# The first slot's sources worked out from one expert's ranks, gathered ahead of the other slots, in a fused attention and mixture-of-experts kernel

## The chip, the cores and the metric

One core of one Trainium2 chip. The metric is the device time of one execution in microseconds; lower is better. All times inside the kernel are microseconds from the first instruction of the profiled execution.

## The reference

Three stages, each feeding the next.

```python
# 1: attention, 2 batches x 8 heads, 768 rows, 64 columns; a row sees the columns of its own hash bucket
mask = q_bucket[:, :, :, None] == k_bucket[:, :, None, :]
scores = np.where(mask, scale * q @ k.T, -1e9);  attn = softmax(scores) @ v
x = attn.transpose(0, 2, 1, 3).reshape(1536, 512)
# 2: top-1 mixture of 8 experts, 512 -> 1024 -> 512
e_idx = np.argmax(x @ w_gate, axis=1)
gate_w = probs[np.arange(N), e_idx];  eom = sigmoid(x @ w_output_gate)
for e in range(8):
    ye = relu(x[e_idx == e] @ w1[e]) @ w2[e]
    out[e_idx == e] = gate_w * eom[:, e] * ye
# 3: dense layer, 512 -> 2048 -> 512, with ELU between
h = x @ w_in;  g = where(h > 0, h, exp(min(h, 0)) - 1);  return g @ w_out
```

## The kernel before

Attention comes first; its rows x are stored to DRAM (`x_rows`). Then the 1536 tokens are sorted by expert into 19 **slots** of 128 rows; every expert's rows start at a slot boundary. For each slot GpSimd gathers 128 rows of x with one indirect DMA (`gather_x`, 256 KB), TensorE turns them (`turn_x`), and runs layer 1, a turn of the hidden rows (`turn_h`) and layer 2 with the expert's weights. Stage 3 follows.

Each engine has its own list of instructions, written out by hand; semaphores tie the lists together. On the vector engine `then(...)` makes the next instruction wait for the one in it. What matters here is the stretch from the end of attention (about 243 us) to layer 1 of slot 1 (263 us):

- **Ranks.** TensorE sums the one-hot matrix of the experts into `ring[0]` (`s_rank`). The ranks are each token's place within its expert, and the counts of all experts.
- **Places.** The vector engine turns ranks into a row number for each token (`c_up`, `c_full`, `s_cum`, `r_b`, `r_at`, `r_tile`, `r_low`), then into two one-hot tensors: `place` (which slot) and `at_row` (which of the 128 rows; three instructions of 4 tiles each, L1048).
- **Sources.** Twelve matmuls of `at_row` and `place` (L1426) give the token number of every row of every slot (`s_token`). The vector engine copies them to `src` (L1054, `s_src`), and GpSimd starts the gathers (L607).
- **Slot table and gates.** The vector engine then works out `slot_tab` (which expert and which of two weight buffers a slot uses: L1055 to L1062, `s_tab`) and the gates' values (L1065 to L1073, `s_parts`). GpSimd multiplies these into `place_g` (L618), for 12 matmuls that TensorE runs behind layer 1 of slot 0 (`gates()`, L1500).
- **Slot 0.** TensorE reads `slot_tab` twice (`expert(0)`), turns the rows of slot 0 (L1441), the scalar and the vector engine copy them (`copy_xt(0)`), and layer 1 runs (L1475).
- **Row numbers.** Behind `copy_xt(0)` the vector engine works out `row_at` and `out_row` (L1144 to L1160). Only then does its loop over the slots begin: `relu(0)` (L1100), `copy_xt(1)` (L1091), and so on.
- **TensorE behind layer 1 of slot 0:** `gates()`, `expert(1)`, `turn_x(1)`, `turn_h(0)` (L1450, waits for `relu(0)`), layer 1 of slot 1.
- **Filling.** `warm(i)` runs WARM[i] matmuls of 512 columns without a use (L1401), so that TensorE is not idle while it waits.
- **Weights.** Expert 1's weights (8 transfers of 512 KB, SyncE, L500) are issued when the rows of slot 0 have landed (`s_xld[0]`). The scalar engine rounds them (L756) and GpSimd works out the low parts (`w_lo`, L518). GpSimd's list is: gathers 0 to 3, the two `place_g`, gathers 4 and 5, then in turn one `w_lo(1, c)` and one gather, eight times.

## Time and profile before

| what | value |
|---|---|
| median of 3 runs (lowest, highest) | 769.1 us (768.97, 769.7) |
| the profiled execution's own time | 769.18 us |
| its span, first to last instruction | 767.4 us |
| TensorE busy | 755.5 us, 98% of the span |
| VectorE, ScalarE, GpSimd busy | 423.9, 345.1, 368.6 us |
| mean granted TensorE clock | 0.997 of full speed |

The span is 1.78 us shorter than the execution's own time. TensorE is busy for nearly all of it, but busy also covers the filling matmuls, so what counts is when real work starts.

### The profile page before, as it was taken

The page shows a single profiled execution, that of the slowest core. Times are in us where ns is not written, and L with a number is a line of the kernel's source. Part 1 is how long each engine was busy: PE and PEld are TensorE (multiplying, and loading weights), DVE is VectorE, ACT ScalarE, POOL GpSimd, SP SyncE. Part 2 cuts the span into 40 slices and gives each one's busy share as a digit, 9 for nine tenths or more (in the row PEclk, how much of TensorE's full clock was granted, in tenths as well). Part 3 has the DMA queues.
Part 4 walks back from the last instruction along what each step waited for, and adds up shares of the span by engine and source line. Part 5 has one row for each costly group of instructions (what it writes and reads, how often), then busy time and mean ns, then how long its engine had stood idle before and what let it go on. Part 6 is the DMA issues. An engine that isn't in the chain of part 4 may idle for free.

```text
span 767.4 us, 12551 instructions
## 1 busy us (share of the span) xinstructions
PE 755.5 (98%) x4247; PEld 631.2 (82%) x4247; DVE 423.9 (55%) x844; ACT 345.1 (45%) x656; POOL 368.6 (48%) x253
## 2 busy tenths in 40 slices
PE   8899999999999999999999999999999999999996
PEld 7677777777776788888888888998899889989985
DVE  8777777777765645454444445588147126414710
ACT  7766677777764214432244210185047117404610
POOL 4776567878720799777987870244200120010001
PEclk9999999999999999999999999999999999999998
DMA  4534323212111867655675610520100010000000
GB/s 100 123 111 107 105 76 94 68 49 67 27 46 26 295 227 261 208 190 166 224 237 164 239 55 28 185 105 1 57 26 1 28 56 1 0 28 15 1 14 28
DMA packets 42781, 73.70 MB, mean 96 GB/s; under 512 B 20352, under 2 KB 24096, under 8 KB 42720
## 3 DMA queue, kind: packets, MB, share of 16 engines
q1 hardware_dynamic: 29632, 30.05, 13.4%
q10 hardware_dynamic: 9584, 31.53, 12.4%
q0 software_dynamic: 3504, 11.30, 4.5%
q8 instruction: 38, 0.62, 0.3%
q14 instruction: 23, 0.19, 0.1%
HBM read 60.48 MB, written 11.28 MB: 94 GB/s over the span
## 4 chain that ended last, share of the span: by engine, by line
PE 62%; issue 29%; POOL 4%; DVE 2%; ACT 1%; DMA 1%; SPq 0%; POOLq 0%; DVEq 0%
PE pair_s L1475 14%; PE pair_t L1490 14%; PE pair_u L1282 8%; PE bank_b L1297 8%; PE pair_s L1269 5%; PE pair_t L1269 4%; PE pair_u L1450 2%; PE bank_b L1321 1%; POOL out L646 1%; PE pair_s L1528 1%; DVE g_lo L1211 1%; PE pair_s L1401 1%; PE bank_a L1238 1%; POOL y_raw L640 1%; POOL w_part L518 1%
## 5 line engine op out<-in xcount | busy, mean ns | idle before, releaser
L518 POOL TENSOR_TENSOR w_part<-w_raw,w_part 128x1024 fp32r<-128x1024 f32 x80 | 190.3, 2405 | 57.5 <-ACT w_part L756 57.3
L756 ACT ACTIVATE w_part<-w_raw 128x1024 fp32r<-128x1024 f32 x72 | 73.7, 1054 | 125.4 <-PE pair_t L1490 99.8
L1577 PE MATMUL pair_t<-w_part,g_hi 128*128 128x512 f32 x384 | 119.0, 391 | 0.3 <-POOL w_part L518 0.3
L646 POOL DMA_INDIRECT out<-o_sb,token x12 | 11.8, 986 | 208.5 <-DVE o_sb L1181 208.5
L1475 PE MATMUL pair_s<-w_part,xs_t 128*128 x456 | 108.8, 394 | 0.2 <-issue 0.2
L1490 PE MATMUL pair_t<-w_part,hid_t 128*128 x456 | 109.0, 394 | 0.0
L1475 PEld LDWEIGHTS pair_s<-w_part,xs_t 128*128 128x128 f32 x456 | 84.3, 188 | 17.7 <-issue 0.9
L1490 PEld LDWEIGHTS pair_t<-w_part,hid_t 128*128 128x128 f32 x456 | 84.4, 188 | 16.8
L855 ACT ACTIVATE elu<-elu 128x384 f32<-128x384 f32 x64 | 33.6, 525 | 124.3 <-DVE elu L1201 124.1
L698 ACT ACTIVATE exps<-exps,nmax 128x768 f32<-128x768 f32 x96 | 88.5, 926 | 1.1 <-DVE exps L912 1.0
L1282 PEld LDWEIGHTS pair_u<-first,exps 128*128 128x128 f32 x564 | 64.3, 140 | 24.2 <-issue 19.0
L1577 PEld LDWEIGHTS pair_t<-w_part,g_hi 128*128 128x128 f32 x384 | 71.6, 188 | 15.1 <-issue 0.7
L1282 PE MATMUL pair_u<-first,exps 128*128 128x128 f32 x564 | 80.7, 277 | 1.8 <-ACT exps_t L706 0.9
L941 DVE COPY exps_t<-pair_u 128x384 f32<-128x384 f32 x94 | 52.1, 554 | 42.6 <-PE pair_u L1282 42.3
L1577 PE MATMUL pair_t<-w_part,g_lo 128*128 128x512 f32 x192 | 74.9, 390 | 0.0
L706 ACT ACTIVATE exps_t<-pair_u 128x384 f32<-128x384 f32 x94 | 45.9, 488 | 59.9 <-PE pair_u L1282 59.3
L1528 PE MATMUL pair_u<-y_t,w_part 128*128 128x384 f32 x384 | 69.3, 334 | 0.3 <-DVE elu L1206 0.3
L1528 PE MATMUL pair_s<-y_t,w_part 128*128 128x384 f32 x384 | 69.3, 335 | 0.0
L1528 PEld LDWEIGHTS pair_u<-y_t,w_part 128*128 128x128 f32 x384 | 66.8, 188 | 0.7 <-DVE elu L1206 0.6
L1528 PEld LDWEIGHTS pair_s<-y_t,w_part 128*128 128x128 f32 x384 | 66.9, 188 | 0.2
L1109 DVE CAST hid_t<-pair_u 128x512 fp32r<-128x512 f32 x38 | 26.0, 685 | 67.2 <-PE pair_u L1450 67.2
L1297 PE MATMUL bank_b<-exps_t,v_nat 128*64 128x384 f32 x336 | 60.4, 495 | 0.0
(219 smaller groups left out, 1091.8 us busy)
## 6 DMA issues: line engine op xcount, KB each, us to landing
w_raw<-in_moe_w ACTq DMA_DIRECT2D x48, 512.0 KB, 6.3
w_raw<-in_moe_w SPq DMA_DIRECT2D x16, 512.0 KB, 5.8
ys_sorted<-ys SPq DMA_DIRECT2D x19, 256.5 KB, 3.7
w_raw<-in_moe_w_in ACTq DMA_DIRECT2D x8, 512.0 KB, 5.2
raw<-in_q SPq DMA_DIRECT2D x16, 192.0 KB, 3.2
raw<-in_k SPq DMA_DIRECT2D x16, 192.0 KB, 3.4
v_nat<-in_v SPq DMA_DIRECT2D x16, 192.0 KB, 2.6
x_rows<-rows_sb SPq DMA_DIRECT2D x32, 96.0 KB, 2.4
```

What stands on the lines that cost most here:

```text
L518: pool.tensor_tensor(chunk_of(w_part, n, 1, c), w_raw[n % 2][c][:, :], chunk_of(w_part, n, 0, c).bitcast(F32), ALU.subtract).then_inc(s_wl ...
L698: act.activation(exps[:, m % 4, :], exps[:, m % 4, :], ACT.Exp, scale=-1.0, bias=nmax[:, g % 2, qt:qt + 1], accum_out=den[:, u % 4, qt:qt ...
L706: act.activation(turned_tile(m, slice(0, JH)), exps_pair(m)[:, 0, 0:HALF].rearrange("p (j n) -> p j n", j=JH), ACT.Copy).then_inc(s_t0, 1)
L756: act.activation(chunk_of(w_part, n, 0, c), w_raw[n % 2][c][:, :], ACT.Copy).then_inc(s_whi, 1)
L941: dve.tensor_copy(turned_tile(m, slice(JH, J)), exps_pair(m)[:, 1, 0:HALF].rearrange("p (j n) -> p j n", j=JH)).then_inc(s_t1, 1)
L1269: mm = pe.matmul(score_pair[m % 2][:, h, 0:HALF], a[rows, g % 3, t], b[rows, g % 3, h * HALF:(h + 1) * HALF], start=first, stop=not first)
L1282: mm = pe.transpose(exps_pair(m)[:, part, n * P:(n + 1) * P], exps[:, m % 4, kt * P:(kt + 1) * P], ident)
L1297: mm = pe.matmul(u_bank(u)[o * D:(o + 1) * D, 0:HALF], v_nat[:, (u - 1 + o) % 4, j, :], turned_half(2 * u - 1 + o)[:, j], start=j == 0, st ...
L1475: mm = pe.matmul(pair_s[:, h, :], xs_t[:, xp, c * P:(c + 1) * P], w_part[:, bass.ds(par, 1), wp, a:a + 512], start=c == 0 and xp == 0 and ...
L1490: mm = pe.matmul(pair_t[:, s % 2, :], hid_t[:, hp, c * P:(c + 1) * P], w_part[:, bass.ds(par, 1), wp, a:a + DM], start=c == 0 and n == 0, ...
L1528: mm = pe.matmul(hidden_bank[n % 4][:, 0:NB], w_in_p[:, wp, c, f * P:(f + 1) * P], y_t[:, yp, c, :], start=c == 0 and m == 0, stop=c == CD ...
L1577: mm = pe.matmul(pair_t[:, t % 2, :], gp[:, f, j * P:(j + 1) * P], w_out_p[:, wp, f, :], start=f == 0 and m == 0, stop=f == FT - 1 and m == 2)
```

## The change

A second way to the sources is added for slot 0, which belongs to expert 0 whatever the data are. `r_first` is the rank within expert 0, less 1024 for tokens of that expert. Compared with a constant row `lowered` (0 to 127, less 1024), it gives `at_row` for slot 0 alone. Twelve matmuls with the token numbers (`row_two`, made on the scalar engine) give the first column of `src`, and gather 0 waits for that (`s_srcf`) and not for `s_src`. The way of before follows, for all slots; the block between `e_cmp` and the second `gate_part` (L1055 to L1073) is moved word for word. The slot table and the gates' arithmetic stand behind `copy_xt(0)`. TensorE no longer reads the slot table for slot 0: its expert and its buffer are constants. The filling matmuls are 10, 4, 12, 3 in place of 10, 14, 16, 3.

```diff
-WARM = (10, 14, 16, 3)
+WARM = (10, 4, 12, 3)
+APART = 1024.0
+    put("lowered", np.arange(P) - APART)
@@ gpsimd
-            pool.wait_ge(s_src, 1)
+            pool.wait_ge(s_srcf, 1)
             for i in range(2):
                 pool.wait_ge(s_xst[i], 16 * HEADS)
-            for s in range(FIRST_SLOTS):
+            gather_x(0)
+            pool.wait_ge(s_src, 1)
+            for s in range(1, FIRST_SLOTS):
                 gather_x(s)
@@ scalar
             act.activation(r_z[:, :], r_z[:, :], ACT.Exp, scale=-1.0).then_inc(s_rb, 1)
+            act.activation(row_two[:, :, :], cc("row").unsqueeze(2).broadcast_to([P, TILES, 2]), ACT.Copy).then_inc(s_two, 1)
@@ vector
+            then(dve.scalar_tensor_tensor(r_first[:, :], oh[:, :, 0], -APART, rank[:, 0:TILES, 0], ALU.mult, ALU.add))
+            for t in range(0, TILES, AT):
+                dve.tensor_tensor(at_row[:, t:t + AT, :], cc("lowered").unsqueeze(1).broadcast_to([P, AT, P]),
+                                  r_first[:, t:t + AT].unsqueeze(2).broadcast_to([P, AT, P]),
+                                  ALU.is_equal).then_inc(s_atf, 1)
             then(dve.tensor_scalar(c_up[:, :], rank[:, TILES, :], 1.0, float(P - 1), ALU.max, ALU.add))
...
+            dve.wait_ge(s_first, 1)
+            dve.tensor_copy(src[:, 0:1], ring[2][:, 0:1]).then_inc(s_srcf, 1)
...
             dve.wait_ge(s_token, 1)
-            dve.tensor_copy(src[:, :], ring[1][:, 0:SLOTS]).then_inc(s_src, 1)
+            dve.tensor_copy(src[:, 1:SLOTS], ring[1][:, 1:SLOTS]).then_inc(s_src, 1)
-            then(dve.tensor_tensor(e_cmp[:, :, :], s_cum[:, 1:E].unsqueeze(1).broadcast_to([P, SLOTS, E - 1]),
...
-            dve.tensor_tensor(gate_part[:, 1, :], gate[:, :], gate_part[:, 0, :].bitcast(F32),
-                              ALU.subtract).then_inc(s_parts, 1)
...
             copy_xt(0)
+
+            then(dve.tensor_tensor(e_cmp[:, :, :], s_cum[:, 1:E].unsqueeze(1).broadcast_to([P, SLOTS, E - 1]),
...
+            dve.tensor_tensor(gate_part[:, 1, :], gate[:, :], gate_part[:, 0, :].bitcast(F32),
+                              ALU.subtract).then_inc(s_parts, 1)
@@ tensor
             warm(1)
+            pe.wait_ge(s_two, 1)
+            for t in range(TILES):
+                if t % AT == 0:
+                    pe.wait_ge(s_atf, t // AT + 1)
+                mm = pe.matmul(ring[2][:, 0:2], at_row[:, t, :], row_two[:, t, :], start=t == 0, stop=t == TILES - 1)
+                if t % AT == AT - 1 and t < TILES - 1:
+                    pe.matmul(pair_s[:, 0, 0:P], w_part[:, 0, 1, 0:P], w_part[:, 0, 0, 0:P], start=True, stop=True)
+            mm.then_inc(s_first, 1)
+            warm(2)
...
-            warm(2)
-            pe.wait_ge(s_tab, 1)
             pe.wait_ge(s_cnt, 1)
             pe.wait_ge(s_src, 1)
-            of = {0: expert(0)}
+            of = {0: (0, NC1, NCH)}
             turn_x(0)
             warm(3)
...
                 if s == 0:
                     gates()
+                    pe.wait_ge(s_tab, 1)
```

On the vector engine, right behind the wait for the ranks, this stood before (the first rows of the chain that ends in `r_low`):

```order
L1030 TENSOR_SCALAR c_up<-bank_a 128x8 [waits s_rank]
L1031 TENSOR_SCALAR c_full<-c_up 128x8 [waits s_dd]
L1032 SCALAR_TENSOR_TENSOR s_cum<-cst,c_full 128x8 [waits s_dd]
L1033 TENSOR_TENSOR r_b<-s_cum,bank_a 128x96 [waits s_dd]
L1035 TENSOR_TENSOR r_b<-r_b,onehot 128x96 [waits s_dd]
```

And this stands there now:

```order
L1038 SCALAR_TENSOR_TENSOR r_first<-onehot,bank_a 128x12 [waits s_rank]
L1040 TENSOR_TENSOR at_row<-cst,r_first 128x512 [waits s_dd]
L1040 TENSOR_TENSOR at_row<-cst,r_first 128x512 x2
L1043 TENSOR_SCALAR c_up<-bank_a 128x8
L1044 TENSOR_SCALAR c_full<-c_up 128x8 [waits s_dd]
L1045 SCALAR_TENSOR_TENSOR s_cum<-cst,c_full 128x8 [waits s_dd]
L1047 CAST src<-pair_u 128x1 [waits s_first,s_dd]
L1048 TENSOR_TENSOR r_b<-s_cum,bank_a 128x96
```

So the old chain from `r_b` on stands behind five added instructions and a wait for TensorE. On the same engine, behind the wait for the sources of all slots, this stood before:

```order
L1054 CAST src<-bank_b 128x19 [waits s_token]
L1055 TENSOR_TENSOR e_cmp<-s_cum,cst 128x133
L1057 TENSOR_TENSOR e_alt<-e_cmp,cst 128x133 [waits s_dd]
L1059 TENSOR_REDUCE tab_f<-e_alt 128x19 [waits s_dd]
L1060 TENSOR_REDUCE tab_f<-e_cmp 128x19
L1061 TENSOR_SCALAR tab_f<-s_cum 128x8
L1062 CAST slot_tab<-tab_f 128x46 [waits s_dd]
L1065 TENSOR_REDUCE r_p<-r_a 128x12 [waits s_rb]
```

And this stands there now:

```order
L1069 CAST src<-bank_b 128x18 [waits s_token]
L1076 CAST xs_t<-bank_b 128x256 [waits s_xt]
L1078 TENSOR_TENSOR xs_t<-bank_a,xs_t 128x256 [waits s_xta]
L1081 TENSOR_TENSOR xs_t<-bank_b,xs_t 128x256 [waits s_xte]
L1136 TENSOR_TENSOR e_cmp<-s_cum,cst 128x133
L1138 TENSOR_TENSOR e_alt<-e_cmp,cst 128x133 [waits s_dd]
L1140 TENSOR_REDUCE tab_f<-e_alt 128x19 [waits s_dd]
```

The 14 instructions from `e_cmp` to the second `gate_part` now stand between `copy_xt(0)` and `c_end`, the first of the 13 that work out the row numbers; `relu(0)` still stands behind those. On TensorE, from the last group of matmuls that give the sources, this stood before:

```order
L1426 MATMUL bank_b<-place,at_row 128x20 [waits s_at,s_place]
L1426 MATMUL bank_b<-place,at_row 128x20 x3
L1401 MATMUL pair_s<-w_part 128x512 x16
L1455 TENSOR_LOAD slot_tab [waits s_src,s_cnt,s_tab]
L1455 ISA x2
L1456 TENSOR_LOAD slot_tab
L1456 ISA x2
L1441 MATMUL bank_a<-first,xs_raw 128x128 [waits s_xld0]
```

And this stands there now:

```order
L1449 MATMUL bank_b<-place,at_row 128x20 [waits s_at,s_place]
L1449 MATMUL bank_b<-place,at_row 128x20 x3
L1464 MATMUL bank_a<-first,xs_raw 128x128 [waits s_xld0,s_src,s_cnt]
L1464 MATMUL bank_a<-first,xs_raw 128x128
L1464 MATMUL bank_b<-first,xs_raw 128x128 x2
L1415 MATMUL pair_s<-w_part 128x512 x3
```

The turn of slot 0's rows now stands right behind those matmuls, and still waits for the sources of all slots, since it writes over the bank that they are read from.

## Rows read from the trace of the kernel before

**Rows 1.** Busy time by stretch (from:to, length, busy of each engine, granted clock, DMA)
```profile
252.00:253.00 1.00, 0.82 (x4) 0.36 (x2) 0.73 (x4) 0.00 (x0) 0.78 (x1) 1.00 0.67 176
...
270.00:480.00 210.00, 210.00 (x1025) 177.18 (x1024) 100.76 (x155) 59.03 (x59) 157.47 (x75) 1.00 0.54 180
```
**Rows 2.** The chain that ended last, slot 0 (start, length, what)
```profile
249.55 3.47 DMA xs_raw<-x_rows,src
...
253.06 0.51 PE bank_a L1441 x2
...
254.59 5.75 PE pair_s L1475 x24
```
**Rows 3.** Timeline of DVE, ranks to sources (start, length, [idle before])
```profile
243.93 0.17 DVE L1030 TENSOR_SCALAR c_up<-bank_a 128x8 uint32<-128x8 f32 x1 [0.15 <-PE bank_a L1410]
...
244.55 0.26 DVE L1033 TENSOR_TENSOR r_b<-s_cum,bank_a 128x96 f32<-128x96 f32 x1
...
246.43 1.89 DVE L1048 TENSOR_TENSOR at_row<-cst,r_low 128x512 fp32r<-128x512 f32 x3
...
249.09 0.18 DVE L1054 CAST src<-bank_b 128x19 uint32<-128x19 f32 x1 [0.69 <-PE bank_b L1426]
```
**Rows 4.** Timeline of PE, the last group of source matmuls
```profile
248.46 0.58 PE L1426 MATMUL bank_b<-place,at_row 128*128 128x20 f32 x4
```
**Rows 5.** Timeline of DVE, from the sources to the copies of slot 1
```profile
249.18 0.29 DVE L1055 TENSOR_TENSOR e_cmp<-s_cum,cst 128x133 f32<-128x133 f32 x1
...
252.66 0.17 DVE L1073 TENSOR_TENSOR gate_part<-gate,gate_part 128x12 fp32r<-128x12 f32 x1
...
254.61 0.41 DVE L1088 TENSOR_TENSOR xs_t<-bank_b,xs_t 128x256 fp32r<-128x256 f32 x1
...
255.13 0.48 DVE L1145 TENSOR_TENSOR pad<-c_full,counts 128x8 f32<-128x8 uint32 x1
...
258.05 0.18 DVE L1160 TENSOR_TENSOR out_row<-part_f,tile_f 128x19 uint32<-128x19 f32 x1
...
260.45 1.22 DVE L1100 TENSOR_SCALAR hid<-pair_s 128x1024 f32<-128x1024 f32 x1 [2.22 <-PE pair_s L1475]
...
262.29 0.69 DVE L1091 CAST xs_t<-bank_b 128x512 fp32r<-128x512 f32 x1 [0.61 <-PE bank_b L1441]
```
**Rows 6.** Timeline of PE, behind layer 1 of slot 0
```profile
260.18 1.41 PE L1500 MATMUL pair_t<-place_g,at_row 128*128 128x40 f32 x12
261.43 0.75 PE L1441 MATMUL bank_b<-first,xs_raw 128*128 128x128 f32 x4
262.02 1.05 PE L1450 MATMUL pair_u<-first,hid 128*128 128x128 f32 x8
263.23 5.75 PE L1475 MATMUL pair_s<-w_part,xs_t 128*128 x24 [0.17 <-issue]
```
**Rows 7.** Timeline of PE, the same place one slot later
```profile
274.78 1.05 PE L1450 MATMUL pair_u<-first,hid 128*128 128x128 f32 x8
275.59 5.72 PE L1475 MATMUL pair_s<-w_part,xs_t 128*128 x24
```
**Rows 8.** Timeline of POOL: gather 0, place_g, first and fourth low part
```profile
249.55 1.09 POOL L607 DMA_INDIRECT xs_raw<-x_rows,src  x1 [14.60 <-DVE src L1054]
...
254.44 1.15 POOL L618 TENSOR_TENSOR place_g<-in_slot,gate_part 128x240 fp32r<-128x240 f32 x2
...
260.01 2.38 POOL L518 TENSOR_TENSOR w_part<-w_raw,w_part 128x1024 fp32r<-128x1024 f32 x1 [1.99 <-ACT w_part L756]
...
270.62 2.41 POOL L518 TENSOR_TENSOR w_part<-w_raw,w_part 128x1024 fp32r<-128x1024 f32 x1
```
**Rows 9.** DMA issues, us to landing: of 252 to 253, then 253.6 to 254.5
```profile
xs_raw<-x_rows,src POOLq DMA_INDIRECT x1, 5.6
...
xs_raw<-x_rows,src POOLq DMA_INDIRECT x1, 8.7
```
**Rows 10.** Timeline of SyncE's queue: expert 1's weights
```profile
253.09 4.78 SPq L500 DMA_DIRECT2D w_raw<-in_moe_w  x8
```

More of the change, by code:

```diff
@@ L92 @@
            ("twice", D), ("rev", TILES * E), ("slot", SLOTS * (E - 1)), ("starts", TILES * COLS),
-           ("alt", SLOTS * (E - 1)), ("iota", P), ("row", TILES)]
+           ("alt", SLOTS * (E - 1)), ("iota", P), ("lowered", P), ("row", TILES)]
 COL = {}
@@ L204, in program @@
             r_low = sb("r_low", [P, TILES])
+            r_first = sb("r_first", [P, TILES])
+            row_two = sb("row_two", [P, TILES, 2], F32R)
             lg_part = sb("lg_part", [P, J, 2 * E])
@@ L339, in program @@
         s_src = sem("s_src")
+        s_atf, s_first, s_srcf, s_two = sem("s_atf"), sem("s_first"), sem("s_srcf"), sem("s_two")
         s_wld = [sem(f"s_wld{c}") for c in range(NCH)]
@@ L1053, in _ @@
             dve.wait_ge(s_token, 1)
-            dve.tensor_copy(src[:, :], ring[1][:, 0:SLOTS]).then_inc(s_src, 1)
-            then(dve.tensor_tensor(e_cmp[:, :, :], s_cum[:, 1:E].unsqueeze(1).broadcast_to([P, SLOTS, E - 1]),
-                                   cc("slot").rearrange("p (s e) -> p s e", e=E - 1), ALU.is_le))
-            then(dve.tensor_tensor(e_alt[:, :, :], e_cmp[:, :, :],
-                                   cc("alt").rearrange("p (s e) -> p s e", e=E - 1), ALU.mult))
-            dve.tensor_reduce(tab_f[:, 0:SLOTS], e_alt[:, :, :], AX.X, ALU.add)
-            dve.tensor_reduce(tab_f[:, SLOTS:2 * SLOTS], e_cmp[:, :, :], AX.X, ALU.add)
-            then(dve.tensor_scalar(tab_f[:, 2 * SLOTS:], s_cum[:, 1:E + 1], 1.0 / P, 1.0, ALU.mult, ALU.add))
-            dve.tensor_copy(slot_tab[:, :], tab_f[:, :]).then_inc(s_tab, 1)
-            dve.wait_ge(s_rb, 1)
-            then(dve.tensor_reduce(r_p[:, :], r_a[:, :, :], AX.X, ALU.add))
-            then(dve.tensor_scalar(r_p[:, :], r_p[:, :], EPS, None, ALU.add))
-            then(dve.reciprocal(r_p[:, :], r_p[:, :]))
-            dve.wait_ge(s_rb, 2)
-            then(dve.tensor_scalar(r_z[:, :], r_z[:, :], 1.0, None, ALU.add))
-            then(dve.reciprocal(r_z[:, :], r_z[:, :]))
-            then(dve.tensor_tensor(gate[:, :], r_p[:, :], r_z[:, :], ALU.mult))
-            then(dve.tensor_copy(gate_part[:, 0, :], gate[:, :]))
-            dve.tensor_tensor(gate_part[:, 1, :], gate[:, :], gate_part[:, 0, :].bitcast(F32),
-                              ALU.subtract).then_inc(s_parts, 1)
+            dve.tensor_copy(src[:, 1:SLOTS], ring[1][:, 1:SLOTS]).then_inc(s_src, 1)
             def copy_xt(s):
@@ L1141, in _ @@
             copy_xt(0)
+            then(dve.tensor_tensor(e_cmp[:, :, :], s_cum[:, 1:E].unsqueeze(1).broadcast_to([P, SLOTS, E - 1]),
+                                   cc("slot").rearrange("p (s e) -> p s e", e=E - 1), ALU.is_le))
+            then(dve.tensor_tensor(e_alt[:, :, :], e_cmp[:, :, :],
+                                   cc("alt").rearrange("p (s e) -> p s e", e=E - 1), ALU.mult))
+            dve.tensor_reduce(tab_f[:, 0:SLOTS], e_alt[:, :, :], AX.X, ALU.add)
+            dve.tensor_reduce(tab_f[:, SLOTS:2 * SLOTS], e_cmp[:, :, :], AX.X, ALU.add)
+            then(dve.tensor_scalar(tab_f[:, 2 * SLOTS:], s_cum[:, 1:E + 1], 1.0 / P, 1.0, ALU.mult, ALU.add))
+            dve.tensor_copy(slot_tab[:, :], tab_f[:, :]).then_inc(s_tab, 1)
+            dve.wait_ge(s_rb, 1)
+            then(dve.tensor_reduce(r_p[:, :], r_a[:, :, :], AX.X, ALU.add))
+            then(dve.tensor_scalar(r_p[:, :], r_p[:, :], EPS, None, ALU.add))
+            then(dve.reciprocal(r_p[:, :], r_p[:, :]))
+            dve.wait_ge(s_rb, 2)
+            then(dve.tensor_scalar(r_z[:, :], r_z[:, :], 1.0, None, ALU.add))
+            then(dve.reciprocal(r_z[:, :], r_z[:, :]))
+            then(dve.tensor_tensor(gate[:, :], r_p[:, :], r_z[:, :], ALU.mult))
+            then(dve.tensor_copy(gate_part[:, 0, :], gate[:, :]))
+            dve.tensor_tensor(gate_part[:, 1, :], gate[:, :], gate_part[:, 0, :].bitcast(F32),
+                              ALU.subtract).then_inc(s_parts, 1)
             dve.wait_ge(s_cnt, 1)
```

## The prediction

> **What bounds the kernel now.** I read the busy time by stretch first. From 270 to 480 us TensorE is busy for the whole 210.00 us at full clock [rows 1]: from slot 1 on nothing makes it wait, so whatever moves the start of that stretch moves the end by as much. The question is only when TensorE begins layer 1 of slot 1, at 263.23 us [rows 6].
>
> The chain that ended last names what holds the stretch ahead of it. Gather 0 leaves at 249.55 us and takes 3.47 us to land; TensorE turns the rows at 253.06 us, 0.04 us after they are there, and layer 1 of slot 0 starts at 254.59 us [rows 2]. TensorE looks busy then, but with filling matmuls. Gather 0 waits for the sources, copied at 249.09 us, and those for a chain on the vector engine that starts with the ranks at 243.93 us [rows 3].
>
> The timelines of the vector engine and TensorE show the stretch up to slot 1. The vector engine has the slot table and the gates at 249.18 to 252.83 us (3.65 us, inside the gather's flight), and from its last copy of slot 0, L1088 at 254.61 us, to the end of L1160 at 258.23 us another 3.62 us. Then it stands idle 2.22 us until layer 1 ends, and starts `relu(0)` at 260.45 us [rows 5]. TensorE has the gates' matmuls, turns slot 1's rows at 261.43 us, the hidden rows at 262.02 us, and starts layer 1 at 263.23 us [rows 6]. From the turn of the hidden rows to the next layer 1 is 1.21 us here and 0.81 us one slot later [rows 7]: 0.40 us are a wait for L1091, which ends at 262.98 us [rows 5].
>
> **The change, step by step.**
>
> *The way for slot 0.* `r_first` is one more chained instruction of 12 elements; its like, three from 243.93 to 244.55 us, take 0.21 us each [rows 3]. The three new `at_row` have the shape of L1048: 1.89 us [rows 3]. They end at 243.93 + 0.21 + 1.89 = 246.03 us. In the way of before the last four matmuls ended 0.72 us after `at_row` (249.04 against 248.32 us) [rows 3, 4]; two columns in place of twenty cost between nothing and as much, and I take as much: 246.75 us. `c_up` to `s_cum` fill 0.62 us of that, so the vector engine waits 0.1 us. It copies column 0 at 246.80 us, against 249.09 us. The stores of x are not in the way: the gather waited for `src` alone [rows 8]. Gather 0 leaves 2.29 us earlier and lands at about 250.73 us. Making `row_two` on the scalar engine is priced by no row here; it lies beside the 2 us of `at_row`.
>
> *The way for all slots.* It is pushed back by what was put ahead of it: `r_b` stood at 244.55 us and comes at 246.89 us (0.09 us behind the copy, as L1055 behind L1054 [rows 3, 5]), 2.34 us later. The sources of all slots are copied at 251.43 to 251.61 us. The turn of slot 0's rows still waits for them. **So the gather is no longer what comes last; the pushed-back chain is.** With 0.14 us from the vector engine to TensorE (248.32 to 248.46 us [rows 3, 4]) the turn starts at 251.75 us: 1.31 us earlier than 253.06 us. Layer 1 of slot 0 moves from 254.59 to 253.28 us and ends at 259.03 us. The two reads of the slot table that are gone lay behind the wait for the gather; I count nothing for them. Queued behind the new waits are, on TensorE, 12 filling matmuls, which end before the sources come, and on GpSimd gathers 1 to 3, 0.9 us later than before.
>
> *The moved block.* It leaves a place where the gather's flight hid it and comes to one where layer 1 of slot 0 hides it, if it fits. L1088 starts at 254.61 - 1.31 = 253.30 us. Behind it stand 3.62 us as before and the block's 3.65 us: `relu(0)` can start at 260.57 us. Layer 1 ends at 259.03 us. The old slack of 2.22 us is 1.43 us too short for a block of 3.65 us, and this eats the 1.31 us: `relu(0)` starts about when it did (260.45 us). It ends at 261.79 us, and the turn of the hidden rows starts at about 261.95 us against 262.02 us. TensorE now stands still before it for about a microsecond, since its turn of slot 1's rows is over at 260.9 us.
>
> *What is left.* With slot 1's rows turned that early, their copy L1091 follows `relu(0)` at once and ends near 262.5 us. The wait of 0.40 us before layer 1 of slot 1 goes: it starts 0.81 us behind the turn of the hidden rows, at 262.76 us. That is 0.47 us earlier.
>
> *Two instructions at a time on VectorE and GpSimd.* L1145 works on 8 elements and takes 0.48 us, where L1160 with 19 takes 0.18 us; it ended at 255.61 us, as `place_g` did on GpSimd at 255.59 us [rows 5, 8]. So 0.30 us of the 3.62 us are a wait for GpSimd. In the new order `place_g` waits for the moved block and runs exactly beside the row numbers' arithmetic, which has several instructions with two inputs from SBUF. The cost is between nothing (0.30 us less than before) and the whole 1.15 us of the two `place_g` (0.85 us more) [rows 8]. I take 0.15 us more, nearer to the row. The Trainium skill (SBUF — State Buffer, "Who interferes with whom") says that a VectorE instruction with two SBUF inputs contends with a GpSimd instruction that reads SBUF, and that the one that started first holds the ports for its whole length. The trace agrees in L1145; by the rule taken strictly, the sum would be near the upper end just given.
>
> *Sum.* -0.07 us (turn of the hidden rows) - 0.40 us (wait that goes) + 0.15 us = -0.3 us. The profiled execution took 769.18 us, 0.08 us over the median of the runs; 769.1 - 0.3 = 768.8 us.
>
> **What is hidden.** GpSimd starts `place_g` at about 257.4 us and not 254.44 us, is through at 258.6 us, and TensorE wants it at 259.0 us or somewhat earlier; were it late by 1 us, TensorE's wait for `relu(0)` would still cover it. Behind come two gathers, of 1.09 us and some 0.2 us between, and then `w_lo(1, 0)` at 261.2 us in place of 260.01 us: 1.2 us later. Layer 1 of slot 2, the first of expert 1, needs four of them; the fourth ended at 270.62 + 2.41 = 273.03 us [rows 8] and would end at 274.2 us, against a start of that layer at 275.59 us [rows 7], or 275.1 us with the gain. This cover of 0.9 us is gone if the vector engine's block runs a microsecond longer, and then it costs what it exceeds it by.
>
> **The rivals.**
>
> *The gain passes whole.* If `relu(0)` were ready by 259.1 us, layer 1 of slot 1 would start 1.31 us earlier: 767.8 us. It needs the vector engine's 7.27 us between L1088 and `relu(0)` to shrink by 1.4 us. Against it: these are the block's own measured lengths, and no more than 0.3 us of waiting in the 3.62 us is seen in the rows. Partial shrinking is likelier.
>
> *Contention at its upper end.* `place_g` holds up the row numbers for 0.85 us more: +0.4 us, 769.5 us.
>
> *Gather 1 comes late; the slower side.* It leaves at 251.61 + 0.28 = 251.9 us. Expert 1's weights, 4 MB, used to be issued at 253.09 us [rows 10], behind gather 1; now they are issued when gather 0 lands, at 250.8 us, ahead of it. The gather issued at 252.22 us took 5.6 us, one among the weights 8.7 us [rows 9]. By these gather 1 lands between 257.5 and 260.6 us, and TensorE wants it at 260.1 us. It decides only beyond 261.2 us, since the turn of the hidden rows waits until 261.95 us. With a landing after 10.7 us the turn of slot 1's rows would start at 262.7 us and layer 1 of slot 1 at 264.2 us: +1.0 us, 770.1 us.
>
> *Slot 0 does not start earlier.* The added way costs more than the 2.34 us, as by 1.3 us, and the turn of slot 0's rows stands where it did. Then `relu(0)` comes 1.3 us later than forecast: 770.1 us. Against it: every added step has its like in rows 3.
>
> **How the numbers follow.** Forecast (between 0.8 us less and 0.1 us more): 0.66. Gain whole: 0.12. Contention: 0.10. Gather 1 late: 0.07. No earlier start: 0.05. The likeliest is 768.8 us. The range goes from the whole gain to most of the way to the two slow cases: 767.7 to 769.9 us. A measurement of this kernel can tell about 0.2%, 1.54 us. Faster than 767.56 us needs more than the whole gain: 0.05. Slower than 770.64 us needs a slow case beyond its price: 0.04. Within: 0.91.
>
> **What would show it.** Gather 0 issued near 247.3 us, the turn of slot 0's rows near 251.8 us right behind the copy of the sources and not the landing, and the granted clock 1.00 there, as it is where TensorE was busy 0.82 of a microsecond [rows 1]. `relu(0)` near 260.6 us with the vector engine never idle before it, TensorE idle about 1 us before the turn of the hidden rows, no wait before layer 1 of slot 1, which starts at 262.8 to 263.1 us. A vector engine that is idle before `relu(0)` would prove me wrong on the main step; TensorE waiting for the DMA of slot 1's rows, on the gather.

## The result, and the profile after

The changed kernel takes 773.08 us in the median of 5 runs (772.4 to 773.61), the kernel before 769.1 us (768.97 to 769.7, 5 runs): ratio 1.005, 95% interval 1.004 to 1.0061. It is slower by about 4 us. The profiled execution took 772.98 us, with a span of 771.2 us against 767.4 us.

The vector engine from the ranks to `relu(0)`, as a timeline (start, length, line, operation, [idle before]); it answers to [rows 3] and [rows 5]:

```profile
243.77 0.17 DVE L1038 SCALAR_TENSOR_TENSOR r_first<-onehot,bank_a 128x12 f32<-128x12 bf16 x1 [0.15 <-PE bank_a L1424]
...
246.64 0.16 DVE L1047 CAST src<-pair_u 128x1 uint32<-128x1 f32 x1 [0.27 <-PE pair_u L1436]
...
251.24 0.17 DVE L1069 CAST src<-bank_b 128x18 uint32<-128x18 f32 x1 [0.69 <-PE bank_b L1449]
...
253.50 0.29 DVE L1136 TENSOR_TENSOR e_cmp<-s_cum,cst 128x133 f32<-128x133 f32 x1
...
256.58 0.17 DVE L1154 TENSOR_TENSOR gate_part<-gate,gate_part 128x12 fp32r<-128x12 f32 x1
...
256.88 0.58 DVE L1159 TENSOR_TENSOR pad<-c_full,counts 128x8 f32<-128x8 uint32 x1
257.49 0.61 DVE L1160 TENSOR_TENSOR past<-cst,c_end 128x96 f32<-128x96 f32 x1
...
259.54 0.18 DVE L1171 CAST tile_f<-tile_no 128x19 f32<-128x19 uint32 x1
259.75 3.05 DVE L1172 SCALAR_TENSOR_TENSOR part_f<-part_f,tile_f 128x19 f32<-128x19 f32 x1
262.83 0.17 DVE L1173 TENSOR_SCALAR tile_f<-tile_f 128x19 f32<-128x19 f32 x1
263.04 0.18 DVE L1174 TENSOR_TENSOR out_row<-part_f,tile_f 128x19 uint32<-128x19 f32 x1
263.25 1.22 DVE L1093 TENSOR_SCALAR hid<-pair_s 128x1024 f32<-128x1024 f32 x1
```

Down to L1171 it runs as forecast or a little ahead; the ranks were there at 243.77 us and not at 243.93 us, so 0.16 us of that lead is not the change's. Then one instruction of 19 elements, L1172, takes 3.05 us where its neighbours take 0.18 us. `relu(0)` (L1093) stands behind it and starts at 263.25 us, not at 260.45 us as before [rows 5]. GpSimd at the same time, against [rows 8]:

```profile
247.08 1.14 POOL L612 DMA_INDIRECT xs_raw<-x_rows,src  x1 [12.29 <-DVE src L1047]
...
256.84 1.15 POOL L625 TENSOR_TENSOR place_g<-in_slot,gate_part 128x240 fp32r<-128x240 f32 x2 [1.68 <-DVE gate_part L1154]
...
259.42 0.95 POOL L612 DMA_INDIRECT xs_raw<-x_rows,src  x1 [0.30 <-issue]
260.39 2.37 POOL L523 TENSOR_TENSOR w_part<-w_raw,w_part 128x1024 fp32r<-128x1024 f32 x1
```

L1172 ends at 262.80 us, 0.04 us after the first low part, `w_lo(1, 0)` (L523), at 262.76 us. In the kernel before, that low part began at 260.01 us, when the row numbers had been over since 258.23 us [rows 5, 8]: the two never met. TensorE's timeline, against [rows 6] and [rows 2]:

```profile
251.52 0.48 PE L1464 MATMUL bank_a<-first,xs_raw 128*128 128x128 f32 x2 [0.32 <-issue]
...
253.46 6.52 PE L1498 MATMUL pair_s<-w_part,xs_t 128*128 128x512 f32 x24
259.81 1.41 PE L1523 MATMUL pair_t<-place_g,at_row 128*128 128x40 f32 x12
261.07 0.75 PE L1464 MATMUL bank_b<-first,xs_raw 128*128 128x128 f32 x4
264.53 1.16 PE L1473 MATMUL pair_u<-first,hid 128*128 128x128 f32 x8 [2.72 <-DVE hid L1093]
265.45 7.34 PE L1498 MATMUL pair_s<-w_part,xs_t 128*128 x24
```

The turn of slot 0's rows is 1.54 us earlier than before, and the turn of the hidden rows 2.51 us later, after a wait of 2.72 us for `relu(0)`. Layer 1 of slot 1 then takes 7.34 us in place of 5.75 us. The reason stands in the busy times by stretch (from:to, length, busy of each engine, granted clock, DMA share, GB/s), against [rows 1]:

```profile
252.00:253.00 1.00, 1.00 (x4) 0.84 (x4) 0.58 (x2) 0.38 (x1) 0.69 (x2) 0.50 0.70 217
...
260.00:264.00 4.00, 1.81 (x15) 1.62 (x15) 3.90 (x4) 2.12 (x2) 3.80 (x4) 1.00 1.03 407
...
265.00:266.00 1.00, 1.00 (x9) 0.91 (x8) 0.93 (x4) 0.86 (x1) 1.00 (x1) 0.80 1.01 414
266.00:269.00 3.00, 3.00 (x9) 2.32 (x8) 2.61 (x4) 2.12 (x2) 2.82 (x3) 0.50 0.65 242
...
270.00:480.00 210.00, 210.00 (x1024) 177.12 (x1023) 100.38 (x153) 56.91 (x56) 157.78 (x75) 1.00 0.54 178
```

TensorE was busy 1.81 of 4 us from 260 to 264 us, and from 266 to 269 us its granted clock is 0.50: 1.2 GHz in place of 2.4 GHz. A first fall stands at 252 us, where TensorE is recorded as busy all the time. From 270 us on there is no wait, as before. So the loss is whole by then: layer 1 of slot 1 starts 2.2 us late and takes 1.6 us longer, which is the 3.8 us of the spans.

### The profile page after: what moved, and what is told of

It reads as the page before. It is cut to its first block, busy times and chain, and to the rows that moved or that the text cites. A ratio compares the mean times of both kernels' runs of the same rounds, so it can differ in the third digit from the quotient of the medians.

```text
span 771.2 us, 12520 instructions
## 1 busy us (share of the span) xinstructions
PE 757.0 (98%) x4247; PEld 632.8 (82%) x4247; DVE 428.6 (56%) x849; ACT 345.2 (45%) x657; POOL 368.5 (48%) x253
## 4 chain that ended last, share of the span: by engine, by line
PE 61%; issue 29%; DVE 4%; POOL 4%; ACT 1%; DMA 1%; SPq 0%; POOLq 0%; DVEq 0%
PE pair_t L1513 14%; PE pair_s L1498 13%; PE pair_u L1296 8%; PE bank_b L1311 8%; PE pair_s L1283 4%; PE pair_t L1283 4%; PE pair_u L1473 2%; PE bank_b L1335 1%; POOL out L653 1%; PE pair_s L1549 1%; DVE g_lo L1225 1%; PE pair_s L1415 1%; PE bank_a L1252 1%; POOL y_raw L647 1%; POOL w_part L523 1%
## 5 line engine op out<-in xcount | busy, mean ns | idle before, releaser
L523 POOL TENSOR_TENSOR w_part<-w_raw,w_part 128x1024 fp32r<-128x1024 f32 x80 | 190.1, 2401 | 59.1 <-ACT w_part L763 58.9
L1498 PE MATMUL pair_s<-w_part,xs_t 128*128 (+1 forms) x456 | 111.2, 401 | 0.0
L1513 PE MATMUL pair_t<-w_part,hid_t 128*128 (+1 forms) x456 | 109.0, 395 | 0.0
L1498 PEld LDWEIGHTS pair_s<-w_part,xs_t 128*128 128x128 f32 x456 | 86.3, 192 | 17.7
```

What stands on the lines that cost most here:

```text
L523: pool.tensor_tensor(chunk_of(w_part, n, 1, c), w_raw[n % 2][c][:, :], chunk_of(w_part, n, 0, c).bitcast(F32), ALU.subtract).then_inc(s_wl ...
L1498: mm = pe.matmul(pair_s[:, h, :], xs_t[:, xp, c * P:(c + 1) * P], w_part[:, bass.ds(par, 1), wp, a:a + 512], start=c == 0 and xp == 0 and ...
L1513: mm = pe.matmul(pair_t[:, s % 2, :], hid_t[:, hp, c * P:(c + 1) * P], w_part[:, bass.ds(par, 1), wp, a:a + DM], start=c == 0 and n == 0, ...
```

## The experiments

All kernels here compute the whole reference. The theory was the **hold** (theory L): L1172 is kept from ending by the first low part, and the wait that follows lets the clock fall. The rivals were the clock alone (theory C), a slow L1172 for a reason of its own (theory O), the length of the moved block itself, and the added way for slot 0. Each diff is against the changed kernel where the text names no other, and shows the lines that matter; a line of dots stands for what is left out. e1 to e12 are the names of the experiments.

**The low part behind the row numbers** (e1). `w_lo(1, 0)` waits for `out_row`; a copy of one element signals it.

```diff
+            pool.wait_ge(s_outrow, 1)
             for c in range(NCH):
                 w_lo(1, c)
```

> The changed kernel, with one wait more: GpSimd begins the first low part of expert 1's weights only when the vector engine has written out_row. In the changed kernel L1172, a scalar_tensor_tensor of 19 elements with two inputs from SBUF, took 3.05 us and ended at 262.80 us, 0.04 us after that low part (260.39 to 262.76 us) ended on GpSimd. Theory L (VectorE was held up by GpSimd's low part, 2.7 us of the 3.8 us lost): L1172 takes about 0.2 us, relu(0) starts at 260.4 to 260.7 us in place of 263.25 us, TensorE waits under 1 us before the turn of the hidden rows, and the time is 769 to 770.5 us. Theory C (TensorE's clock is what costs: it fell to half in 252 to 255 us and in 265 to 269 us): the two falls stay, at least the first, and the time stays above 771 us even if relu(0) is early. Theory O (L1172 is slow for a reason of its own, its place in the program or its data): it takes 3 us again, and the time stays at 773 us.

Measured: 769.03 us, ratio to the kernel before 1.0003 (0.9994 to 1.0013). The vector engine's timeline of this kernel:

```profile
259.75 0.18 DVE L1174 SCALAR_TENSOR_TENSOR part_f<-part_f,tile_f 128x19 f32<-128x19 f32 x1
259.97 0.40 DVE L1175 TENSOR_SCALAR tile_f<-tile_f 128x19 f32<-128x19 f32 x1
260.40 0.18 DVE L1177 TENSOR_TENSOR out_row<-part_f,tile_f 128x19 uint32<-128x19 f32 x1
...
260.68 1.22 DVE L1095 TENSOR_SCALAR hid<-pair_s 128x1024 f32<-128x1024 f32 x1
```

The same instruction at the same 259.75 us takes 0.18 us, so it is not slow by itself. The low part begins at 260.85 us. Layer 1 of slot 1 starts at 263.09 us. The whole 4.05 us between the changed kernel and this one come from the low part's place. The first fall of the clock was there too (0.59 from 252 to 256 us), so it isn't part of the loss.

**The row numbers of the output later** (e2). `part_row` to `out_row` stand behind `copy_ht(0)`.

```diff
-            then(dve.tensor_scalar(part_row[:, :], src[:, :], P - 1, None, ALU.bitwise_and))
...
                 copy_ht(s)
+                if s == 0:
+                    out_rows()
```

> The changed kernel, with the seven instructions from part_row to out_row behind copy_ht(0), so that only c_end to row_at stand ahead of relu(0). Theory L: relu(0) is no longer behind the held instruction and starts when layer 1 of slot 0 ends, 259.1 to 260.0 us; layer 1 of slot 1 starts at 262.0 to 262.6 us, and the seven instructions may each be held by a low part further on, beside TensorE's work, without a cost. Time 768 to 769.5 us, 767.5 to 768 us if the clock does not fall. Theory C: relu(0) is early, but the clock still falls in 252 to 255 us, which costs about 1 us: 769 to 770 us. Theory O (the slow instruction is slow anywhere): a 3 us instruction stands behind copy_ht(0), where it costs nothing, so the same times as by L; only its length tells them apart, if it does not lie beside a low part.

Measured: 769.26 us, ratio 1.0003 (0.9993 to 1.0012). `relu(0)` starts at 258.67 us and layer 1 of slot 1 at 261.79 us, 1.44 us earlier than before [rows 6]. But the moved instructions now meet the second, third and fourth low part:

```profile
265.05 1.17 DVE L1169 TENSOR_SCALAR part_row<-src 128x19 uint32<-128x19 uint32 x1
...
266.67 3.09 DVE L1172 CAST tile_f<-tile_no 128x19 f32<-128x19 uint32 x1
...
270.22 3.09 DVE L1175 TENSOR_TENSOR out_row<-part_f,tile_f 128x19 uint32<-128x19 f32 x1
```

The low parts run from 263.76 to 266.17 us, 267.31 to 269.72 us and 270.85 to 273.27 us, and each held instruction ends within 0.05 us of one. `relu(1)` stands behind all three and starts at 273.35 us, and TensorE waits 1.2 us for it. So the hold goes with the pair of instructions that meet, not with the place in the program.

**The moved block alone** (e3; the diff is against the kernel before). The kernel before, with the block behind `copy_xt(0)` and slot 0's constants, without the way for slot 0.

```diff
             copy_xt(0)
+            then(dve.tensor_tensor(e_cmp[:, :, :], s_cum[:, 1:E].unsqueeze(1).broadcast_to([P, SLOTS, E - 1]),
...
-            of = {0: expert(0)}
+            of = {0: (0, NC1, NCH)}
```

> The kernel before, with one part of the change alone: the slot table and the gates' arithmetic behind copy_xt(0), and TensorE's constants for slot 0. No second way for slot 0, the fillings as before (10, 14, 16, 3). L1088 stays at 254.6 us, and behind it stand 3.62 + 3.65 us: relu(0) at 261.9 us if nothing holds the vector engine, 1.4 us later than before; with it layer 1 of slot 1 starts 1.0 to 1.3 us later: 770.1 to 770.5 us. Theory L: an instruction of the row numbers may be caught beside a low part or a gather of GpSimd again; each caught costs up to 2.4 us: 770.5 to 773 us. Theory C: with the old fillings the clock does not fall before slot 0 (PEclk 1.00 in 252 to 255 us); a second fall behind a long wait would show a granted clock of 0.5 in 264 to 270 us.

Measured: 774.52 us, ratio 1.0075 (1.0058 to 1.0091). The hold is there (3.03 us from 261.24 us, low part from 261.87 us), TensorE waits 4.0 us, and the clock falls to 0.70 from 264 to 268 us.

**The moved block alone, low part behind the row numbers** (e6). The diff is against e3; `out_row` signals `s_outrow`.

```diff
+            pool.wait_ge(s_outrow, 1)
             for c in range(NCH):
                 w_lo(1, c)
```

> The kernel before with the moved block alone, as in the run at 774.5 us, and GpSimd's first low part of expert 1 behind out_row. Theory L: the 3.03 us of L1158 become about 0.2 us, relu(0) starts at about 262.0 us in place of 264.7 us, TensorE waits about 1.2 us and not 4.0 us, the clock does not fall, and layer 1 of slot 1 starts at about 264.3 us, 1.1 us later than before: 770.2 us (770 to 771). The rest over the kernel before is the block itself. If the hold were not what cost in that run, the time stays over 773 us.

Measured: 770.08 us, ratio 1.0013 (1.0004 to 1.0022); TensorE waits 1.3 us and the clock stays at 1.00. So of the 5.4 us of e3 about 1 us is the block's own length in its new place, and 4.4 us are the hold and the clock.

**The way for slot 0 alone** (e4). The changed kernel, with the block in front of `copy_xt(0)`.

```diff
             dve.tensor_copy(src[:, 1:SLOTS], ring[1][:, 1:SLOTS]).then_inc(s_src, 1)
+            then(dve.tensor_tensor(e_cmp[:, :, :], s_cum[:, 1:E].unsqueeze(1).broadcast_to([P, SLOTS, E - 1]),
...
             copy_xt(0)
```

> The changed kernel, with the slot table and the gates' arithmetic back where they were, ahead of copy_xt(0); the second way for slot 0 and the fillings 10, 4, 12, 3 stay. The sources are copied at 251.4 us, the block ends at 255.1 us, so the copies of slot 0 come 2.6 us later than in the changed kernel, layer 1 of slot 0 starts at about 256.0 us (1.4 us later than before), and relu(0) is ready for it. Theory L: no instruction of the vector engine of over 1 us before relu(0); time 770 to 771 us with a full clock. Theory C: the clock falls near 252 us in this kernel too, since the sparse matmuls ahead are the same, and costs 0.8 to 1.5 us more: 771 to 772.5 us.

Measured: 774.52 us, ratio 1.0066 (1.004 to 1.0091). I had expected no hold, and this failed: two instructions are held, by two low parts. The vector engine, and then GpSimd:

```profile
258.52 2.97 DVE L1171 CAST tile_f<-tile_no 128x19 f32<-128x19 uint32 x1
...
261.95 3.06 DVE L1174 TENSOR_TENSOR out_row<-part_f,tile_f 128x19 uint32<-128x19 f32 x1
```

```profile
259.04 2.41 POOL L523 TENSOR_TENSOR w_part<-w_raw,w_part 128x1024 fp32r<-128x1024 f32 x1
...
262.59 2.38 POOL L523 TENSOR_TENSOR w_part<-w_raw,w_part 128x1024 fp32r<-128x1024 f32 x1
```

GpSimd, done with `place_g` sooner, begins its low parts sooner (259.04 us in place of 260.01 us), since expert 1's weights come sooner: they are issued at 250.93 us in place of 253.09 us, and the first low part no longer waits for the scalar engine's rounding [rows 8, 10]. Either half of the change brings the row numbers and the low parts together: the block by pushing the first back, the way for slot 0 by pulling the second forward, and here the row numbers are 1.25 us later as well (`part_row` at 257.86 us in place of 256.61 us). The holds aren't the whole of this kernel's loss: its layer 1 of slot 0 waits for the copies and starts at 255.52 us, 0.93 us later than before, and the clock is at 0.51 from 252 to 256 us and at 0.72 from 264 to 268 us.

**The wait filled** (e5). The changed kernel, with 10 filling matmuls of 512 columns in front of the turn of slot 0's hidden rows. It tells the clock from the wait.

```diff
+                if s == 0:
+                    for i in range(10):
+                        pe.matmul(pair_t[:, 0, :], w_part[:, 0, 1, 0:P], w_part[:, 0, 0, 0:512], start=True, stop=True)
                 if s < SLOTS:
                     turn_h(s)
```

> The changed kernel, with ten filling matmuls of 512 columns on TensorE between the turn of slot 1's rows and the turn of slot 0's hidden rows, where it waited 2.7 us for relu(0). The vector engine's held instruction stays. If the wait is what lets the clock fall behind it (granted clock 0.5 in 265 to 269 us of the changed kernel, where layer 1 of slot 1 took 7.3 us), the clock stays at 1.00 there, that layer takes 5.75 us, and the time is about 1.3 us less than the changed kernel's 773.1: 771.5 to 772 us. If the fall has another cause, layer 1 of slot 1 takes 7 us again and the time stays at 773 us.

Measured: 771.45 us, ratio 1.0034 (1.0022 to 1.0046). The hold is unchanged (3.06 us). Its stretches:

```profile
252.00:256.00 4.00, 4.00 (x14) 3.12 (x13) 3.34 (x14) 1.71 (x3) 2.70 (x3) 0.59 0.94 329
...
264.00:268.00 4.00, 3.81 (x22) 3.10 (x21) 3.86 (x8) 2.46 (x3) 3.83 (x3) 1.00 0.82 331
```

The first fall stays, the second is gone, and layer 1 of slot 1 takes 5.70 us. The second fall is worth 773.08 - 771.45 = 1.6 us, the hold the other 771.45 - 769.03 = 2.4 us.

**Wider fillings between the source matmuls** (e10). The changed kernel, with the four single fillings between the groups (two among the matmuls for slot 0, two among those for all slots) 512 columns wide and not 128. One of the two places:

```diff
-                    pe.matmul(pair_s[:, 0, 0:P], w_part[:, 0, 1, 0:P], w_part[:, 0, 0, 0:P], start=True, stop=True)
+                    pe.matmul(pair_s[:, 0, :], w_part[:, 0, 1, 0:P], w_part[:, 0, 0, 0:512], start=True, stop=True)
```

> The changed kernel, with 512 columns in place of 128 in the four single filling matmuls between the groups of source matmuls. The clock's first fall (granted clock 0.5 in 252 to 255 us) does not come: layer 1 of slot 0 takes 5.7 us and not 6.5 us. The held instruction and the second fall behind it stay. Since relu(0) waits for the vector engine and not for layer 1, the time moves little: 772.5 to 773.5 us by theory L. If the first fall is part of the 4 us lost, it is 771.5 to 772.3 us.

Measured: 772.92 us, ratio 1.0049 (1.0033 to 1.0064). The clock is 1.00 from 252 to 256 us and layer 1 of slot 0 takes 5.72 us, but TensorE only waits longer for `relu(0)`: 4.0 us. The second fall stays. The first fall costs nothing as long as the hold is there.

**The low part in four pieces** (e9). The changed kernel, `w_lo(1, 0)` as four instructions of 256 columns.

```diff
+                    for i in range(4):
+                        at = slice(i * CHUNK // 4, (i + 1) * CHUNK // 4)
+                        done = pool.tensor_tensor(chunk_of(w_part, 1, 1, 0)[:, at], w_raw[1][0][:, at],
+                                                  chunk_of(w_part, 1, 0, 0)[:, at].bitcast(F32), ALU.subtract)
```

> The changed kernel, with the first low part of expert 1's weights (one GpSimd instruction of 1024 columns, 2.38 us) as four instructions of 256 columns. In the changed kernel L1172 on the vector engine took 3.05 us, from 0.3 us into gather 5 to the end of that low part. Theory L, with the hold lasting as long as the GpSimd instruction that is running (and not as long as GpSimd is busy): the instruction is freed after the first piece, 0.6 to 0.7 us instead of 2.38 us, so it takes 1.2 to 1.5 us, and those behind it may each be held for one piece: relu(0) starts at 261.5 to 262.7 us in place of 263.25 us, and the time is 770.5 to 772.5 us. If the vector engine is held as long as GpSimd has work of any kind, L1172 takes 3 us again and the time stays at 773 us. Theory O: the same, 3 us and 773 us.

Measured: 770.39 us, ratio 1.003 (1.0016 to 1.0043). The vector engine, and GpSimd's four pieces:

```profile
259.75 0.79 DVE L1180 SCALAR_TENSOR_TENSOR part_f<-part_f,tile_f 128x19 f32<-128x19 f32 x1
260.58 0.64 DVE L1181 TENSOR_SCALAR tile_f<-tile_f 128x19 f32<-128x19 f32 x1
261.25 0.66 DVE L1182 TENSOR_TENSOR out_row<-part_f,tile_f 128x19 uint32<-128x19 f32 x1
```

```profile
260.37 2.81 POOL L635 TENSOR_TENSOR w_part<-w_raw,w_part 128x256 fp32r<-128x256 f32 x4
```

One hold of 3.05 us became three of 0.64 to 0.79 us, where one piece takes 0.72 us, and `relu(0)` starts at 261.95 us. A hold goes by the GpSimd instruction, not by how long GpSimd has work: that was without a pause from 260.37 to 263.18 us. I had expected the first hold to last until the first piece ends, 1.2 to 1.5 us; it was over at 260.54 us, 0.17 us after that piece's record begins. The Trainium skill (SBUF — State Buffer, "Who interferes with whom") says that the engine that comes second is blocked for the first one's whole instruction; the rows agree on the length. They don't agree on the order: by the records the vector instruction begins first (259.75 us against 260.39 us in the changed kernel), and still it is the one that waits.

**Better versions** (e7, e8, e11, e12). The diff of e7 is against the changed kernel, those of e11 and e12 are against e8. The question was whether the earlier start can reach the end at all. In e7 the first four instructions of the output rows stand right behind the copy of the sources, in idle time, and GpSimd's gathers 4 and 5 and the low parts wait for `out_row`:

```diff
             dve.tensor_copy(src[:, 1:SLOTS], ring[1][:, 1:SLOTS]).then_inc(s_src, 1)
+            dve.wait_ge(s_src, 1)
+            then(dve.tensor_scalar(part_row[:, :], src[:, :], P - 1, None, ALU.bitwise_and))
...
+            pool.wait_ge(s_outrow, 1)
             for s in range(FIRST_SLOTS, NEXT_SLOTS):
                 gather_x(s)
```

> The changed kernel with two edits: the first four of the seven instructions of out_row stand right behind the copy of src, in the 0.9 us in which the vector engine waits for the turn of slot 0's rows; and GpSimd begins gathers 4 and 5 and the first low part only when out_row is written. Theory L: nothing holds the vector engine for more than 0.6 us before relu(0), which starts at 259.0 to 259.6 us; layer 1 of slot 1 starts at 261.8 to 262.2 us, 1.0 to 1.4 us earlier than before, no instruction of the vector engine stands beside a low part afterwards that TensorE waits for, and the gain stays to the end: 767.7 to 768.1 us with a full clock, up to 769.2 us in executions in which the clock falls near 252 us. If the moved start is lost somewhere further on in any case, 769 us.

Measured: 768.75 us, ratio 0.9999 (0.999 to 1.0008), with the clock at 0.58 from 252 to 256 us, layer 1 of slot 0 at 6.91 us and layer 1 of slot 1 from 263.13 us. No instruction is held any more, but I had expected that layer from 261.8 to 262.2 us: `relu(0)` now waits 0.94 us for the slow layer 1 of slot 0. e8 adds the wide fillings of e10:

> The kernel with split rows, and the four single filling matmuls between the groups of source matmuls with 512 columns in place of 128. If the clock falls near 252 us because TensorE had little to stream in 244 to 251 us, it falls in fewer executions or not at all: the median is at or below that of the kernel with split rows, by up to 1 us, and the spread of its times is narrower. The wider fillings may push the sources back by 0.1 to 0.3 us. If the fall has nothing to do with it, the median is 0 to 0.3 us higher and the spread is the same.

Measured: 769.19 us, ratio 1.0005 (0.9996 to 1.0014). The clock stays at 1.00 and layer 1 of slot 1 starts at 262.17 us, 1.06 us earlier than before. The time isn't at or below e7's, as I had expected with the clock up. TensorE's waits show where it is lost:

```profile
PE pair_s L1502 <- POOL w_part L524: 0.9, 1, 0.9
```

Layer 1 of slot 2 waits for the fourth low part of expert 1, which is over at 275.43 us, not at 273.03 us. e11 puts the low parts in front of gathers 4 and 5 and leaves two gathers for the end of the list:

```diff
-            for s in range(FIRST_SLOTS, NEXT_SLOTS):
-                gather_x(s)
...
                 w_lo(1, c)
-                gather_x(NEXT_SLOTS + c)
+                gather_x(FIRST_SLOTS + c)
+            for s in range(FIRST_SLOTS + NCH, NEXT_SLOTS + NCH):
+                gather_x(s)
```

> The kernel with split rows and wide fillings, and with another order on GpSimd: the first low part stands right behind out_row and gathers 4 and 5 go among the low parts (one gather behind each, the last two at the end). In the run with split rows and wide fillings the moved start was lost at slot 2, where TensorE waited 0.9 us for the fourth low part (it ended at 275.5 us, layer 1 of slot 2 was ready at 274.5 us). Here the low parts start 2.2 us earlier, at about 260.2 us, so the fourth ends at about 273.3 us and TensorE does not wait: layer 1 of slot 2 starts at about 274.5 us, 1.1 us earlier than in the kernel before, and the time is 767.8 to 768.2 us. If the gain is lost elsewhere, 769 us.

Measured: 769.23 us, ratio 1.001 (1.0001 to 1.0019). The wait at slot 2 is gone, but expert 2's low parts begin at 290.66 us in place of 288.44 us, and TensorE waits the same 0.9 us at slot 4; of the two times expected, it is the one for a gain that is lost elsewhere. e12 puts gather 4 into GpSimd's idle time ahead of `place_g`, gather 5 behind it, and lets the low parts alone wait for `out_row`:

```diff
-FIRST_SLOTS = 4
+FIRST_SLOTS = 5
...
-            pool.wait_ge(s_outrow, 1)
             for s in range(FIRST_SLOTS, NEXT_SLOTS):
                 gather_x(s)
+            pool.wait_ge(s_outrow, 1)
             for c in range(NCH):
```

> The version with the rows' arithmetic split and wide filling (768.75 and 769.19 us for its two forms) with two more moves on GpSimd: gather 4 stands ahead of place_g, in 1.45 us of idle time, and only the first low part waits for out_row, no longer gathers 4 and 5. If GpSimd's list is what takes the gain back, the first low part starts near 260.3 us in place of 262.4, the fourth is over near 273.2, expert 2's begin near 288.6 as in the kernel before, TensorE waits neither at slot 2 nor at slot 4, layer 1 of slot 1 starts at 262.1 to 262.4 us (263.23 before), and the time is 767.9 to 768.3 us. If the gain is lost at yet another place further on, the time is 769 us again, and that place shows as a wait of TensorE behind slot 4. If gather 5, which now runs beside the row numbers, holds the vector engine as the low part did, relu(0) comes after 261 us and the time is 769.5 us or more.

Measured: 768.2 us (767.91 to 769.1, 11 runs), the kernel before 769.16 us beside it; ratio 0.9989 (0.998 to 0.9998). The timelines of GpSimd and of TensorE:

```profile
259.93 2.38 POOL L524 TENSOR_TENSOR w_part<-w_raw,w_part 128x1024 fp32r<-128x1024 f32 x1 [0.39 <-DVE out_row L1177]
...
270.56 2.41 POOL L524 TENSOR_TENSOR w_part<-w_raw,w_part 128x1024 fp32r<-128x1024 f32 x1
...
288.27 11.86 POOL L524 TENSOR_TENSOR w_part<-w_raw,w_part 128x1024 fp32r<-128x1024 f32 x5
```

```profile
261.16 1.15 PE L1477 MATMUL pair_u<-first,hid 128*128 128x128 f32 x8 [0.17 <-DVE hid L1100]
262.06 5.71 PE L1502 MATMUL pair_s<-w_part,xs_t 128*128 x24
...
274.38 3.00 PE L1502 MATMUL pair_s<-w_part,xs_t 128*128 x12
```

GpSimd's low parts stand where they stood before [rows 8], TensorE waits for none of them, and the 1.17 us won at layer 1 of slot 1 are still 1.2 us in the spans (766.2 against 767.4 us). This version is 4.9 us faster than the changed kernel and 0.96 us (0.1%) faster than the kernel before; the interval for the latter just leaves out 1, and the spans and TensorE's timeline of the two profiled executions say the same. It isn't a time that the kernel before never reaches: of its 79 executions beside the experiments 19 took 767.7 to 768.5 us, though none of the 15 beside e12, and e12 took under 768.5 us in 9 of 11. What makes the kernel before reach it isn't known, since none of those executions was profiled.

## Why the prediction was wrong

The forecast was 768.8 us within 767.7 to 769.9 us. The measured 773.08 us lies outside, on the slower side. One step failed, the price of two engines at a time; a second, the clock behind a longer wait, was not in the sum.

- **The way for slot 0: right.** Column 0 was copied at 246.64 us (forecast 246.80), the gather issued at 247.08 us (247.3), the sources of all slots copied from 251.24 us (251.43), and the turn started at 251.52 us (251.75), right behind the sources. Of the 1.54 us that this is ahead of the kernel before, 0.16 us are the earlier ranks; the rest, 1.38 us, is near the forecast's 1.31 us.
- **The moved block: right in kind, and shorter.** It stood behind `copy_xt(0)` and took from 253.50 to 256.75 us, 3.25 us in place of 3.65 us. Up to 259.75 us the vector engine was ahead of the forecast: with 0.6 us of row numbers left, `relu(0)` would have started near 260.4 us (forecast 260.57 us).
- **"Two instructions at a time on VectorE and GpSimd": the step that failed.** It priced contention with `place_g` alone, between 0.30 us less and 0.85 us more. The meeting with `place_g` stayed inside these bounds, at three times the 0.15 us taken: `pad` and `past` took 0.58 and 0.61 us, 0.45 us more than the same two before (0.48 and 0.26 us). What was at hand was larger. Behind `place_g` and two gathers GpSimd had low parts of 2.38 us each, and the row numbers end in instructions with two inputs from SBUF, the kind that the forecast itself had named; the hold was 3.05 us, where the instruction had taken 0.18 us before.
- **"What is hidden": looked at one side only.** The start of `w_lo(1, 0)` was worked out (261.2 us), but only to ask whether it would be late. It stood 0.6 us behind the end of the row numbers by the forecast's own figures. It came at 260.39 us, 0.8 us earlier: `place_g` started at 256.84 us and not 257.4 us, and the two gathers with their gaps took 2.4 us and not 2.6 us. The holds begin up to 0.64 us ahead of the low part's record, so the 0.6 us were no margin at all. In e1 the low part begins 0.46 us later than in the changed kernel, and 4 us are won; that an error of less than a microsecond decided them is argued from this, since there the low part also waits for `out_row`. A margin that thin belonged among the rivals.
- **The clock: left out of the sum.** The forecast had about 1 us of standing still before the turn of the hidden rows, and no price for a longer one. The wait of 2.72 us was followed by 3 us at 0.50, worth 1.6 us by e5. The clock at 252 us was forecast at 1.00, from a row in which TensorE was busy 0.82 of a microsecond, and was 0.50 with TensorE recorded as busy 1.00 of one: the busy share was no sign of the clock. This cost nothing here (e10), but some 1 us in the start of layer 1 of slot 1 once the hold is gone: 263.13 us in e7, 262.17 us in e8. In the time that microsecond doesn't show, since e8 loses it again at slot 2.
- **What the change is worth without the hold: not shown.** The forecast was a gain of 0.3 us. e1 and e7 can't be told from the kernel before, and their intervals (0.9994 to 1.0013, 0.999 to 1.0008) leave room for that gain and for none. The sum of the loss: 2.4 us of hold and 1.6 us of clock against e1.
- **The rivals.** Gather 1 was in time: TensorE turned slot 1's rows at 261.07 us without waiting for it. The rival in which the added way costs too much didn't come: slot 0 started earlier. The gain passes nearly whole in e12, 1.17 of 1.31 us at slot 1, but only with the row numbers split, the low part behind them, gather 4 moved and wide fillings.

Not told apart: how much each of e12's moves gives in the time, as e7 to e12 differ from each other by less than a microsecond. The two falls of the clock were read in one profiled execution of each kernel.

## What to carry to other kernels

When a block of small vector instructions moves, or the data of a GpSimd instruction comes sooner, lay the timelines of both engines side by side and ask which pairs meet for the first time; the price of a meeting is what is left of the GpSimd instruction, and up to 0.64 us more when its record hasn't begun, not the length of the small one. Work out the start of every long instruction near the moved block with its error, not only whether it is late. And when TensorE starts earlier, follow the slowest supplier (here GpSimd's low parts) to the next places where it hands over, since the gain has to pass each of them.
